# Attention and two gated layers on one core: products of zeros between the first real products, and a first group ordered by units

## The chip, the core and the metric

The kernel runs on one core of one Trainium2 chip. Its engines run side by side and meet at semaphores: PE (TensorE, matmuls and transposes), DVE (VectorE), ACT (ScalarE), POOL (GpSimd) and SP (SyncE, which here issues DMAs). The metric is the device time of one execution in microseconds, lower being better; a comparison takes the median of several executions.

## What is computed

The reference, cut to what matters (batch 2, 8 heads, 768 rows, head size 64):

```python
scores = scale * q @ k.T - slope[h] * dist      # keep: the first n_global=8 keys,
scores = where(keep, scores, -1e9)              #       and the last n_local=96 keys
a = softmax(scores);  x = a @ v                 # x: 2 x 768 x 512
h = relu(x @ w_in);   h = h * sigmoid(conv3(h)); x = h @ w_out
h = relu(x @ w_in2);  u, v = split(h);  v = normalise(v)
out = (u * (w_spatial @ v + b_spatial)) @ w_out2
```

Every matmul runs in 32-bit formats. The weight products behind attention are each made of three products of halves ("hi" and "lo"), which is why PE has so much to do there.

## The kernel before, in words

**Units.** Attention is cut into 48 units. A unit is 128 query rows of one pair of heads; three units of one pair are a triple p (`TG` = 3), four triples are a group (`GU` = 12 units), and there are four groups. Unit u needs, for each of its two heads, scores against 128 or 256 keys (128 for units 0, 3, 6, 9), and passes these steps:

1. PE `scores(p)` (L1426): the scores of the three units of triple p into PSUM; the third unit's are `third_scores`.
2. DVE `bias_scores(u)` (L1028): adds a bias table and takes the row minimum, two instructions of line L1038.
3. ACT `soften(u)` (L707): two exponentials, with the row sums.
4. DVE `invert_sums(u, n)` (L1044): adds a small number and takes the reciprocal, for n units at once (L1047, L1049).
5. POOL `scale_probs(u)` (L614): multiplies both heads' probabilities (L619).
6. PE `turn_probs(u)` (L1453): transposes (L1464).
7. ACT `copy_pt(u)` or DVE `take_pt(u)` (L1051): PSUM to SBUF; `turned_on_dve` (L403) says which.
8. PE `weigh(u)` (L1467): times the values (L1488). After a triple, ACT `round_x` and DVE `rest_of_x` take the result out of its bank, which the next triple's `weigh` waits for.

**Order.** No scheduler is involved: every engine runs its list in the order in which the program writes it. On PE a round is turn (three units), scores of the triple after next, weigh (three units). From triple 4 on, PE also runs the first weight layer of the group before (`f1`, L1509) between the transposes, 24 matmuls a triple. All the engines stand in strict lists, so an instruction whose semaphore is late holds everything behind it.

**What stands around the change.** PE begins with `WARM` = 10 products of a tile of zeros (L1515), then `scores(0)` and `scores(1)`. DVE builds three parts of the bias table on the way (`build_table`, L1013: one long and one short instruction each). Its inversions are made alone for units 0, 1, 2, 5, 8, 11, 14 and by pairs between. POOL also scales queries (L606, L600) and splits the first layer's weights into hi (L628) and lo (L630) in eight pieces (`PIECES_AFTER`).

Of the kernel before, what the change touches and what calls it, by code (L numbers as in the profile page):

```python
# [4 lines left out]
F32 = mybir.dt.float32  # L5
# [7 lines left out]
P = 128  # L13
# [16 lines left out]
WARM = 10  # L30
TW = 5 * P

# [35 lines left out]
PIECES_AFTER = {8: 1, 11: 1, 14: 2, 17: 2, 20: 2}  # L68
# [9 lines left out]
def build_program(nc, q, k0, k1, v0, v1, n_keys, weights, conv_w, b_spatial, out):  # L78
    ctx = ExitStack()
    with ctx:  # L80
# [205 lines left out]
        tables = sem("tables")  # L286
        path_in = sem("path_in")
# [115 lines left out]
        def turned_on_dve(u):  # L403
            return u < GU and (u % TG == 1 or u % TG == 2 and u // TG % 2 == 1)
# [21 lines left out]
        INVERTED_ALONE = (0, 1, 2, 5, 8, 11, 14)  # L426

        def inversion(u):
            if u < TG * (HP + 1):
                return sum(i <= u for i in INVERTED_ALONE) - 1 + sum(i <= u for i in range(TG, TG * (HP + 1), TG))  # L430
            return len(INVERTED_ALONE) + HP + u // TG - (HP + 1)

# [145 lines left out]
        def _(pool):  # L578
# [34 lines left out]

            def scale_probs(u):  # L614
# [26 lines left out]
            pieces = 0  # L641
            for u in range(ALL_UNITS):
# [8 lines left out]
                for _ in range(PIECES_AFTER.get(u, 0)):  # L651
                    split_piece(pieces)
                    pieces += 1
# [43 lines left out]
        def _(act):  # L697
# [88 lines left out]
            soften(0)  # L786
            soften(1)
            copy_pt(0)
            soften(2)
            for p in range(ALL_TRIPLES):  # L790
                u = TG * p
                for tt in range(TG):
                    if p + 1 < ALL_TRIPLES:
                        soften(u + TG + tt)
                    if p >= F1_FIRST and tt == 2:
                        relu_h(2 * (p - F1_FIRST))
                    if u + tt > 0 and not turned_on_dve(u + tt):
                        copy_pt(u + tt)
                    if tt == 0 and p > 0:
                        round_x(p - 1)  # L800
                if p >= F1_FIRST:
                    relu_h(2 * (p - F1_FIRST) + 1)
# [184 lines left out]
        def _(dve):  # L987
# [24 lines left out]

            def build_table(at_col, width):  # L1013
# [136 lines left out]
            build_table(AT_LATER, 2 * P)  # L1150
# [3 lines left out]
            take_pt(1)  # L1154
# [636 lines left out]
```

## Time and profile before

| | us |
|---|---|
| median of 3 runs | 373.0 |
| lowest and highest of them | 372.86, 374.86 |
| the profiled execution, its own time | 373.0 |
| its span, first to last instruction | 371.2 |
| PE busy in the span | 359.6 (97%) |
| DVE, ACT, POOL busy | 215.2, 176.8, 89.5 |

The profiled execution took 373.0 us in all, of which 371.2 us are the span; 1.8 us lie around it. Start times in the timeline count from the start of the span. A row "x12" stands for twelve instructions of one kind that follow each other, with their time together; the bracket behind it is the idle time of that engine just before, and what ended it. A score or weigh matmul of 32-bit data shows as two records, so a `scores` of three units with 12 records has 6 matmul instructions.

### The profile page before, as it was taken

Reading aid. Unit: us, or ns where it says so; the run is one execution under the profiler, and the core shown is the slowest. Engines: PE = TensorE matmul, PEld = TensorE weight load, DVE = VectorE, ACT = ScalarE, POOL = GpSimd, SP = SyncE. Lnnn points to the kernel's source line nnn. Section 1 sums busy time; section 2 is a strip of 40 time slices with the busy share of each in tenths; the row PEclk is TensorE's granted clock in tenths of the full one; section 3 lists DMA queues with packets and bytes.
Section 4 is the critical chain, followed back from the end, with each engine's and each line's share of the span. In section 5 each row is a group of like instructions: output and inputs, shape, how many; then the busy total and the mean of one; then the engine's idle time right before and its main releaser. Section 6 shows DMA issues by size and latency. Waiting matters only on the chain.

```text
span 371.2 us, 6142 instructions
## 1 busy us (share of the span) xinstructions
PE 359.6 (97%) x2266; PEld 326.4 (88%) x2266; DVE 215.2 (58%) x569; ACT 176.8 (48%) x448; POOL 89.5 (24%) x166
## 2 busy tenths in 40 slices
PE   6889999999999999999999999999999999999994
PEld 2557989888998999999989999998899999998883
DVE  6678599767867678779866780214863444440000
ACT  3577776666777579664364640213653111112221
POOL 4659986555443300000030200001400000000000
PEclk9699999999999999999999999999999999999999
DMA  7934332223422305322100000001241000002222
GB/s 223 398 136 128 94 95 78 81 94 96 141 82 63 130 0 171 98 74 64 49 2 0 3 0 0 2 0 45 69 158 58 0 2 0 0 2 86 86 87 91
DMA packets 12085, 27.70 MB, mean 75 GB/s; under 512 B 1552, under 2 KB 3984, under 8 KB 12048
## 3 DMA queue, kind: packets, MB, share of 16 engines
q1 hardware_dynamic: 11760, 27.10, 21.6%
q8 instruction: 20, 0.33, 0.4%
q14 instruction: 17, 0.14, 0.2%
q10 hardware_dynamic: 288, 0.13, 0.2%
HBM read 24.08 MB, written 3.15 MB: 73 GB/s over the span
## 4 chain that ended last, share of the span: by engine, by line
PE 93%; DVE 3%; POOL 1%; issue 1%; ACT 0%; DVEq 0%; POOLq 0%
PE bank L1538 20%; PE bank L1540 20%; PE bank L1539 19%; PE bank L1509 18%; PE bank L1464 6%; PE bank L1488 5%; PE bank L1419 5%; DVE p_sb L1038 1%; PE bank L1515 1%; POOL p_sb L619 1%; DVE pt_sb L1055 1%; DVE xT L1060 0%; POOL q_sb L600 0%; DVE denom L1049 0%; DVE denom L1047 0%
## 5 line engine op out<-in xcount | busy, mean ns | idle before, releaser
L1509 PE MATMUL bank<-xT,w_hi 128*128 128x384 f32 x256 | 69.4, 344 | 0.0
L711 ACT ACTIVATE p_sb<-p_sb,row_min 128x256 f32<-128x256 f32 (+1 forms) x96 | 46.3, 486 | 26.6 <-DVE row_min L1038 26.6
L619 POOL TENSOR_SCALAR p_sb<-p_sb,denom 128x256 f32<-128x256 f32 (+1 forms) x96 | 47.0, 504 | 47.2 <-DVE denom L1049 47.2
L1509 PEld LDWEIGHTS bank<-xT,w_hi 128*128 128x128 f32 x256 | 45.9, 188 | 0.2 <-issue 0.2
L1075 DVE SCALAR_TENSOR_TENSOR c_sb<-h_sb,conv_sb,c_sb 128x382 f32<-128x382 f32 (+1 forms) x64 | 43.0, 672 | 2.3
L1509 PE MATMUL bank<-xT,w_lo 128*128 128x384 f32 x128 | 44.1, 344 | 0.0
L1538 PE MATMUL bank<-g_hi,w_hi 128*128 128x386 f32 (+1 forms) x128 | 43.3, 338 | 0.0
L1540 PE MATMUL bank<-g_hi,w_lo 128*128 128x386 f32 (+1 forms) x128 | 43.2, 337 | 0.0
L1539 PE MATMUL bank<-g_lo,w_hi 128*128 128x386 f32 (+1 forms) x128 | 43.1, 336 | 0.0
L1038 DVE CUSTOM_DVE_ANT_0 p_sb<-bank,table 128x256 f32<-128x256 f32 (+1 forms) x96 | 32.6, 397 | 12.9 <-PE bank L1419 12.5
L635 POOL TENSOR_SCALAR rstd<-mean_var 128x1 f32<-128x1 f32 x12 | 4.5, 374 | 129.3 <-DVE mean_var L1103 129.3
L1464 PE MATMUL bank<-ident,p_sb 128*128 128x128 f32 x176 | 29.9, 286 | 4.1 <-POOL p_sb L619 4.0
L1540 PE MATMUL bank<-w_hi,vn 128*128 128x384 f32 x96 | 32.3, 336 | 0.0
L1538 PE MATMUL bank<-w_hi,vn 128*128 128x384 f32 x96 | 32.3, 336 | 0.0
L1539 PE MATMUL bank<-w_lo,vn 128*128 128x384 f32 x96 | 32.3, 336 | 0.0
L1464 PEld LDWEIGHTS bank<-ident,p_sb 128*128 128x128 f32 x176 | 20.6, 142 | 11.1 <-POOL p_sb L619 5.7
L775 ACT CAST gt<-u_sb 128x384 fp32r<-128x384 f32 x16 | 8.2, 513 | 42.8 <-DVE u_sb L1128 42.8
L719 ACT COPY pt_sb<-bank 128x512 f32<-128x512 f32 (+1 forms) x42 | 22.8, 543 | 7.6 <-PE bank L1464 6.9
L1419 PE MATMUL bank<-k_sb,q_sb 64*128 64x256 f32 (+1 forms) x192 | 25.6, 398 | 0.8 <-DMA k_sb<-in_k 0.6
L751 ACT ACTIVATE x<-bank 128x382 fp32r<-128x382 f32 (+1 forms) x16 | 7.9, 493 | 38.4 <-PE bank L1540 38.2
L1488 PEld LDWEIGHTS bank<-pt_sb,v_sb 128*64 128x64 f32 x352 | 19.2, 138 | 6.1 <-issue 4.8
L1539 PEld LDWEIGHTS bank<-g_lo,w_hi 128*128 128x128 f32 x128 | 24.2, 189 | 0.0
(93 smaller groups left out, 762.6 us busy)
## 6 DMA issues: line engine op xcount, KB each, us to landing
stage<-in_weights SPq DMA_DIRECT2D x17, 512.0 KB, 3.4
v_sb<-in_v SPq DMA_DIRECT2D x8, 390.0 KB, 3.6
k_sb<-in_k SPq DMA_DIRECT2D x8, 384.0 KB, 3.4
out_dram<-out_sb SPq DMA_DIRECT2D x12, 256.0 KB, 2.1
q_sb<-in_q SPq DMA_DIRECT2D x13, 192.0 KB, 2.4
v_sb<-in_v SPq DMA_DIRECT2D x6, 260.0 KB, 3.3
k_sb<-in_k SPq DMA_DIRECT2D x5, 256.0 KB, 2.9
stage_late<-in_weights SPq DMA_DIRECT2D x2, 512.0 KB, 10.7
```

Source lines behind the costliest of these rows:

```text
L619: nc.gpsimd.tensor_scalar(probs_h, probs_h, denom[:, u % SLOTS, h:h + 1], 1.0, ALU.mult, ALU.mult).then_inc(scaled, 1)
L711: nc.scalar.activation(p_sb[:, u % SLOTS, h, 0:n], p_sb[:, u % SLOTS, h, 0:n], ACT.Exp, bias=row_min[:, u % SLOTS, h:h + 1], scale=-1.0, a ...
L719: nc.scalar.copy(pt_sb[:, u % PT_SLOTS, :, 0:n], pt_ps(u)[:, :, 0:n]).then_inc(pt_in, 1)
L1038: nc.vector.tensor_tensor_reduce(out=p_sb[:, u % SLOTS, h, 0:n], in0=score_cols(u, h), in1=table[:, at_col:at_col + n], scale=slope(2 * hp ...
L1075: nc.vector.scalar_tensor_tensor(dst, src, w, dst, ALU.mult, ALU.add).then_inc(tapped, 1)
L1419: return nc.tensor.matmul(score_cols(u, h), queries[rows, tt * P:(tt + 1) * P], keys_t[rows, at_key:at_key + n], start=True, stop=True)
L1464: last = nc.tensor.transpose(pt_ps(u)[:, h, c:c + P], p_sb[:, u % SLOTS, h, c:c + P], ident[:])
L1488: last = nc.tensor.matmul(xt_ps[h * D:(h + 1) * D, tt * P:(tt + 1) * P], rows[:, h * DV:h * DV + D], pt_sb[:, u % PT_SLOTS, h, n * P:(n + ...
L1509: last = nc.tensor.matmul(h_bank(j)[:, 0:C], w, x, start=r == 0, stop=r == F1_GROUP - 1)
L1538: nc.tensor.matmul(ps, a_hi, b_hi, start=start, stop=False)
L1539: nc.tensor.matmul(ps, a_hi, b_lo, start=False, stop=False)
L1540: return nc.tensor.matmul(ps, a_lo, b_hi, start=False, stop=stop)
```

## The change

- **Products of zeros.** `WARM` becomes (8, 3, 6, 4): 8 products before `scores(0)`, 3 before `scores(1)`, 6 behind it, 4 behind the first turn. They write bank 4 and not bank 7.
- **The third table part.** Its long instruction leaves DVE; POOL makes it of two instructions, ahead of its first `scale_probs`, and DVE waits for it (`later_table`).
- **Copies.** In the first group only units 1, 4, 7, 10 are copied by DVE; units 5 and 11 go to ACT.
- **DVE by units.** In units 0 to 14 every inversion is alone. Ahead of the copy of unit u stands the inversion of unit u+2, behind it the biasing of unit u+4.
- **ACT by units.** `soften(2)` comes ahead of `copy_pt(0)`; in the first group `soften(u+3)` stands ahead of `copy_pt(u)` (behind it in triple 0).
- **POOL.** A piece of the weights is split in two steps: the rounding (L628 of before) of pieces 0 and 1 now stands behind units 6 and 9, the rest (L630 of before) still behind units 8 and 11.

```diff
-WARM = 10
+WARM = (8, 3, 6, 4)
+COUNT_STEPS = 5
-PIECES_AFTER = {8: 1, 11: 1, 14: 2, 17: 2, 20: 2}
+ROUND_AFTER = {6: 1, 9: 1, 14: 2, 17: 2, 20: 2}
+REST_AFTER = {8: 1, 11: 1, 14: 2, 17: 2, 20: 2}
...
         def turned_on_dve(u):
-            return u < GU and (u % TG == 1 or u % TG == 2 and u // TG % 2 == 1)
+            return u < GU and u % TG == 1
...
-        INVERTED_ALONE = (0, 1, 2, 5, 8, 11, 14)
+        ALONE = TG * (HP + 1)
...
+            later = table[:, AT_LATER:AT_T0]
+            pool.wait_ge(tables, COUNT_STEPS)
+            nc.gpsimd.tensor_scalar(later, rel[:, AT_LATER:AT_T0], count_f[:, 1:2], 1.0, ALU.is_ge, ALU.mult
+                                    ).then_inc(later_table, 1)
+            pool.wait_ge(later_table, 1)
+            nc.gpsimd.tensor_tensor(later, later, behind[:, AT_LATER:AT_T0], ALU.add).then_inc(later_table, 1)
...
             act.wait_ge(consts, 8)
-            soften(0)
-            soften(1)
-            copy_pt(0)
-            soften(2)
-            for p in range(ALL_TRIPLES):
+            for u in range(TG):
+                soften(u)
+            for u in range(GU):
+                if u < TG and not turned_on_dve(u):
+                    copy_pt(u)
+                soften(u + TG)
+                if u >= TG and not turned_on_dve(u):
+                    copy_pt(u)
+                if u % TG == 0 and u > 0:
+                    round_x(u // TG - 1)
+            for p in range(HP, ALL_TRIPLES):
...
             bias_scores(1)
             invert_sums(0, 1)
-            build_table(AT_LATER, 2 * P)
+            near = table[:, AT_LATER:AT_LATER + GK]
+            dve.wait_ge(later_table, 2)
+            link(nc.vector.tensor_tensor(near, near, reach[:], ALU.min))
             bias_scores(2)
             invert_sums(1, 1)
             bias_scores(3)
-            take_pt(1)
-            invert_sums(2, 1)
-            bias_scores(4)
-            bias_scores(5)
-            invert_sums(3, 2)
-            invert_sums(5, 1)
-            for p in range(1, ALL_TRIPLES + 1):
+            for u in range(GU):
+                invert_sums(u + 2, 1)
+                if turned_on_dve(u):
+                    take_pt(u)
+                if u % TG == 1 and u > TG:
+                    rest_of_x(u // TG - 1)
+                if u + 4 < ALONE:
+                    bias_scores(u + 4)
+            invert_sums(ALONE - 1, 1)
+            for p in range(HP, ALL_TRIPLES + 1):
...
+            def warm(n):
+                for _ in range(n):
+                    nc.tensor.matmul(banks[4][:], zeros[:, 0:P], zeros[:], start=True, stop=True)
+
+            warm(WARM[0])
             scores(0)
+            warm(WARM[1])
             scores(1)
+            warm(WARM[2])
...
                     turn_probs(TG * p + tt)
+                    if p == 0 and tt == 0:
+                        warm(WARM[3])
```

On PE, at the program's start, before (bank<-zeros are the products of zeros, k_sb,q_sb the scores, ident,p_sb the transposes):

```order
L1515 MATMUL bank<-zeros 128x512 x10
L1419 MATMUL bank<-k_sb,q_sb 128x128 x2
L1419 MATMUL bank<-k_sb,q_sb 128x256 x4
L1419 MATMUL bank<-k_sb,q_sb 128x128 x2
L1419 MATMUL bank<-k_sb,q_sb 128x256 x2
L1464 MATMUL bank<-ident,p_sb 128x128 x6
L1419 MATMUL bank<-k_sb,q_sb 128x256 x2
L1464 MATMUL bank<-ident,p_sb 128x128 x4
```

and now, of the same place:

```order
L1541 MATMUL bank<-zeros 128x512 x8
L1444 MATMUL bank<-k_sb,q_sb 128x128 x2
L1444 MATMUL bank<-k_sb,q_sb 128x256 x4
L1541 MATMUL bank<-zeros 128x512 x3
L1444 MATMUL bank<-k_sb,q_sb 128x128 x2
L1444 MATMUL bank<-k_sb,q_sb 128x256 x2
L1541 MATMUL bank<-zeros 128x512 x6
L1489 MATMUL bank<-ident,p_sb 128x128 x2
L1541 MATMUL bank<-zeros 128x512 x4
L1489 MATMUL bank<-ident,p_sb 128x128 x4
L1444 MATMUL bank<-k_sb,q_sb 128x256 x2
L1489 MATMUL bank<-ident,p_sb 128x128 x4
```

The real products keep their order; products of zeros stand in three places between them, 21 in all where there were 10.

On DVE, from the second half of the biasing of unit 3 on, before (a 128x128 or 256 ISA row with p_sb is a biasing, denom rows are an inversion, COPY is `take_pt(1)`):

```order
L1038 ISA p_sb,row_min<-bank,table 128x128
L1038 ISA row_min 128x1
L1055 COPY pt_sb<-bank 128x512
L1047 TENSOR_SCALAR denom<-denom 128x2
L1049 RECIPROCAL denom<-denom 128x2
```

and now:

```order
L1063 ISA p_sb,row_min<-bank,table 128x128
L1063 ISA row_min 128x1
L1072 TENSOR_SCALAR denom<-denom 128x2
L1074 RECIPROCAL denom<-denom 128x2
L1063 ISA p_sb,row_min<-bank,table 128x256
L1063 ISA row_min 128x1
L1063 ISA p_sb,row_min<-bank,table 128x256
L1063 ISA row_min 128x1
L1072 TENSOR_SCALAR denom<-denom 128x2
L1074 RECIPROCAL denom<-denom 128x2
L1080 COPY pt_sb<-bank 128x512
```

The copy of unit 1 now stands behind the inversions of units 2 and 3 and the biasing of unit 4.

On ACT, from its first exponential on, before (COPY is `copy_pt`, of unit 0 and then of unit 2):

```order
L711 ACTIVATE p_sb,denom<-p_sb,row_min 128x128 x2
L711 ACTIVATE p_sb,denom<-p_sb,row_min 128x256 x2
L719 COPY pt_sb<-bank 128x2x128
L711 ACTIVATE p_sb,denom<-p_sb,row_min 128x256 x2
L711 ACTIVATE p_sb,denom<-p_sb,row_min 128x128 x2
```

and now:

```order
L730 ACTIVATE p_sb,denom<-p_sb,row_min 128x128 x2
L730 ACTIVATE p_sb,denom<-p_sb,row_min 128x256 x4
L738 COPY pt_sb<-bank 128x2x128
L730 ACTIVATE p_sb,denom<-p_sb,row_min 128x128 x2
L730 ACTIVATE p_sb,denom<-p_sb,row_min 128x256 x2
```

The exponentials of unit 2 moved ahead of the copy of unit 0.

## Rows read from the trace of the kernel before

**Rows 1.** Page, part 2: PE's granted clock in 40 slices of the span, in tenths

```profile
PEclk9699999999999999999999999999999999999999
```

**Rows 2.** Waits of PE, whole span: us in total, times, longest

```profile
PE bank L1464 <- POOL p_sb L619: 4.0, 5, 1.3
```

**Rows 3.** Stages by windows: length, busy PE, PEld, DVE, ACT, POOL, clock, DMA, GB/s

```profile
0.00:34.50 34.50, 27.88 (x203) 16.89 (x203) 23.70 (x116) 20.13 (x72) 20.93 (x51) 0.90 0.63 222
34.50:371.20 336.70, 331.76 (x2066) 309.49 (x2064) 191.48 (x454) 156.68 (x377) 68.59 (x117) 1.00 0.18 60
```

**Rows 4.** Windows around the fall and rise of the clock

```profile
7.95:11.20 3.25, 0.76 (x4) 0.45 (x4) 2.64 (x16) 2.36 (x10) 1.58 (x4) 1.00 1.04 390
11.30:14.60 3.30, 2.73 (x12) 1.40 (x10) 2.35 (x11) 1.74 (x9) 1.62 (x4) 0.50 1.02 386
14.60:18.00 3.40, 3.40 (x20) 2.27 (x20) 1.20 (x9) 1.65 (x7) 2.80 (x7) 0.50 1.05 415
```

**Rows 5.** Timeline of the first 15 us: start, us, engine, line, instruction

```profile
4.26 0.39 PEld L1515 LDWEIGHTS bank<-zeros 128*128 128x128 bf16 x2 [0.28 <-issue]
...
5.07 1.36 PE L1419 MATMUL bank<-k_sb,q_sb 64*128 64x128 f32 x12
...
7.02 0.93 PE L1419 MATMUL bank<-k_sb,q_sb 64*128 64x128 f32 x8 [0.59 <-DMA k_sb<-in_k]
...
8.43 0.47 DVE L1015 SCALAR_TENSOR_TENSOR table<-rel,count_f,behind 128x256 f32<-128x256 f32 x1
...
8.61 0.87 POOL L619 TENSOR_SCALAR p_sb<-p_sb,denom 128x128 f32<-128x128 f32 x2 [2.64 <-DVE denom L1049]
...
9.28 0.58 PE L1464 MATMUL bank<-ident,p_sb 128*128 128x128 f32 x2 [1.33 <-POOL p_sb L619]
...
10.17 0.51 ACT L711 ACTIVATE p_sb<-p_sb,row_min 128x256 f32<-128x256 f32 x1
...
10.49 0.93 POOL L619 TENSOR_SCALAR p_sb<-p_sb,denom 128x256 f32<-128x256 f32 x2 [1.01 <-DVE denom L1049]
...
11.03 1.14 PE L1464 MATMUL bank<-ident,p_sb 128*128 128x128 f32 x4 [1.16 <-POOL p_sb L619]
...
11.40 0.58 POOL L606 TENSOR_SCALAR q_sb<-q_sb,q_scale 128x384 f32<-128x384 f32 x1
...
12.21 0.69 DVE L1055 COPY pt_sb<-bank 128x512 f32<-128x512 f32 x1 [1.34 <-PE bank L1464]
...
13.89 1.08 PE L1464 MATMUL bank<-ident,p_sb 128*128 128x128 f32 x4 [0.57 <-POOL p_sb L619]
...
14.90 2.51 PE L1419 MATMUL bank<-k_sb,q_sb 64*128 64x128 f32 x12
```

**Rows 6.** Timeline of the rounds behind it, 17 to 35 us

```profile
17.34 1.64 PE L1488 MATMUL bank<-pt_sb,v_sb 128*64 128x128 f32 x20
...
18.91 1.31 PE L1464 MATMUL bank<-ident,p_sb 128*128 128x128 f32 x10
...
21.72 0.55 DVE L1060 TENSOR_TENSOR xT<-bank,xT 128x384 fp32r<-128x384 f32 x1
...
22.32 1.31 PE L1488 MATMUL bank<-pt_sb,v_sb 128*64 128x128 f32 x20 [0.37 <-DVE xT L1060]
...
26.17 1.57 PE L1419 MATMUL bank<-k_sb,q_sb 64*128 64x256 f32 x12
...
26.41 1.28 POOL L630 TENSOR_TENSOR w_lo<-stage,w_hi 128x512 fp32r<-128x512 f32 x1
...
27.66 1.31 PE L1488 MATMUL bank<-pt_sb,v_sb 128*64 128x128 f32 x20
```

**Rows 7.** The last of these rounds, and the end of the stage

```profile
33.24 1.31 PE L1488 MATMUL bank<-pt_sb,v_sb 128*64 128x128 f32 x20
...
34.48 0.66 PE L1464 MATMUL bank<-ident,p_sb 128*128 128x128 f32 x4
```

**Rows 8.** Windows: the round from 27.6 us

```profile
27.60:33.20 5.60, 5.00 (x44) 3.15 (x42) 4.42 (x20) 4.21 (x15) 5.04 (x10) 1.00 0.36 107
```

More of the change, by code:

```diff
@@ L286, in build_program @@
         tables = sem("tables")
+        later_table = sem("later_table")
         path_in = sem("path_in")
@@ L423, in wait_chunk @@
                 eng.wait_ge(chunk_in[n % 2], 16 * (n // 2))
[L426 removed]
+        ALONE = TG * (HP + 1)
         def inversion(u):
[L429 to L431 removed]
+            return u if u < ALONE else ALONE + u // TG - (HP + 1)
         def values_of(u):
@@ L639, in invert_std @@
                                         ALU.pow).then_inc(rstd_in, 1)
-            pieces = 0
+            rounded = split = 0
             for u in range(ALL_UNITS):
@@ L650, in _ @@
                         scale_queries(pg)
-                for _ in range(PIECES_AFTER.get(u, 0)):
-                    split_piece(pieces)
-                    pieces += 1
+                for _ in range(ROUND_AFTER.get(u, 0)):
+                    round_piece(rounded)
+                    rounded += 1
+                for _ in range(REST_AFTER.get(u, 0)):
+                    rest_of_piece(split)
+                    split += 1
             for i in range(B * NT):
@@ L794, in _ @@
                         soften(u + TG + tt)
-                    if p >= F1_FIRST and tt == 2:
+                    if tt == 2:
                         relu_h(2 * (p - F1_FIRST))
-                    if u + tt > 0 and not turned_on_dve(u + tt):
-                        copy_pt(u + tt)
-                    if tt == 0 and p > 0:
+                    copy_pt(u + tt)
+                    if tt == 0:
                         round_x(p - 1)
-                if p >= F1_FIRST:
-                    relu_h(2 * (p - F1_FIRST) + 1)
+                relu_h(2 * (p - F1_FIRST) + 1)
             round_x(ALL_TRIPLES - 1)
@@ L1164, in _ @@
                         bias_scores(u + TG + tt)
-                    if tt > 0 and p < HP and turned_on_dve(u + tt):
-                        take_pt(u + tt)
                 rest_of_x(p - 1)
@@ L1513, in _ @@
             pe.wait_ge(consts, 1)
-            for _ in range(WARM):
-                nc.tensor.matmul(banks[7][:], zeros[:, 0:P], zeros[:], start=True, stop=True)
+            def warm(n):
+                for _ in range(n):
+                    nc.tensor.matmul(banks[4][:], zeros[:, 0:P], zeros[:], start=True, stop=True)
+            warm(WARM[0])
             scores(0)
+            warm(WARM[1])
             scores(1)
+            warm(WARM[2])
             pe.wait_ge(consts, 9)
```

23 lines of the change are left out of this document (12 added, 11 removed).

## Prediction, made before the changed kernel ran

> **What bounds the kernel now.** I began with the windows by stage. From 34.5 us to the end PE is busy 331.76 of 336.70 us; in the 34.5 us before it, 27.88, with a granted clock of 0.90 [rows 3]. The page shows the clock below its level in the second slice alone, apart from the 9 of the first [rows 1]. So there are two kinds of time: 336.7 us that only less work on PE could shorten, and a first stage of 34.5 us with 6.6 us of idle PE and some us at half clock. The list of PE's waits says what the idle time is: 4.0 us in five waits of a transpose for POOL's scaling, the end of the chain scores, bias, exponential, inversion, scaling [rows 2]. The change touches this stage alone, so the question is when PE reaches the point where it no longer waits: the turn of unit 12, at 34.48 us [rows 7]. What arrives earlier there ends earlier.
>
> The clock: between the second scores and 11.2 us PE is busy 0.76 of 3.25 us, the granted clock still 1.00. In the 3.30 us behind it the clock is 0.50, and also in the 3.40 us after those [rows 4]. These are the two levels, 2.4 and 1.2 GHz. The fall follows a stretch in which PE did little: it waited 1.33 us, worked 0.58, waited 1.16 [rows 5]. Half clock shows in the durations: 12 score records take 2.51 us at 14.90 [rows 5] and 1.57 at 26.17, where four of them are longer too [rows 6].
>
> **The start (-0.4 us).** Two products of zeros fewer stand ahead of `scores(0)`. The last two weight loads of zeros take 0.39 us together [rows 5], so `scores(0)` can begin 0.4 us before 5.07. If its operands were late the gain would be 0; I take 0.4. `scores(1)` still begins at 7.02, since a transfer of keys released it [rows 5]. The 3 products ahead of it fit: scores(0) ends 0.4 us before 6.43, and three cost 0.6 us by the pair of 0.39.
>
> **The third table (-0.5 us on DVE's chain).** The 0.47 us at 8.43 leave DVE, between the first inversion and the biasing of unit 2 [rows 5]. POOL gets two instructions. Neither is in the trace; the first is bounded below by a scaling of 256 columns (half of 0.93 for two, 0.47 [rows 5]) and the second lies between half and the whole of the 1.28 us for 512 columns [rows 6]. That is 1.1 to 1.8 us, and POOL has 2.64 us idle just ahead of its first scaling [rows 5]; with the 0.9 us by which that scaling may come earlier, at worst 0.1 us is left. Cost taken: 0. Inversion(1) and so POOL's scaling of unit 1 move from 10.49 to 9.6, by 0.4 + 0.5.
>
> **The products of zeros behind scores(1) and turn(0).** At 0.2 us each, 6 last 1.3 us from 7.02 + 0.8, to 9.1, and turn(0) began at 9.28 [rows 5]. The 4 last 0.85 us behind it: turn(0) at 9.1 takes 0.25, so they end at 10.2; turn(1) can begin at 9.6 + 0.54 = 10.15 (POOL's start to PE's, 10.49 to 11.03 [rows 5]). They fill the gaps and cost 0 to 0.3 us; I take 0. With them PE is busy nearly throughout 7.0 to 10.6, where it had been busy for a quarter. I therefore take the clock at 1.00 throughout.
>
> **Turn(2): from 13.89 to 11.6.** Before, the exponentials of unit 2 began at 10.17, behind a copy that waited for turn(0). Its inversion stood behind `take_pt(1)`, 12.21 to 12.90, which had waited 1.34 us for turn(1) [rows 5]. Both orders are gone. What is late next is POOL: scaling of unit 1 from 9.6 (0.93), scaling of queries (0.58 at 11.40), first half of unit 2 (0.5) [rows 5]: 11.6 us. The inversion is ready before: biasing of unit 2 ends at 9.2, two exponentials of 0.5 and the inversion at 10.6.
>
> **Weigh(0): from 17.34 to 13.5.** Before, 3.45 us from turn(2) to it at half clock (13.89, 14.90, 17.34 [rows 5, 6]). At full clock: turn(2) 0.7, held by POOL's second half (0.46), and 12 score records at half of the spacing 17.34 - 14.90, so 1.2. Sum 11.6 + 0.7 + 1.2 = 13.5. That is 3.8 us gained.
>
> **The three rounds: from 15.90 to 13.7.** From weigh(0) to weigh(9) PE took 33.24 - 17.34 = 15.90 us, in rounds of 4.98, 5.34 and 5.58 [rows 6, 7]. Its own work in a round is 33.24 to 34.48 = 1.24 for weigh [rows 7], 1.31 less the tail for the turn, and 1.49 for scores (26.17 to 27.66 [rows 6]): 4.0 us. After the change the inversions are one unit apart, so the turn is fed early; the late one is the biasing of the round's last unit, which the third scores wait for and which now stands behind `take_pt` and `rest_of_x`. That loop: weigh 1.24, turn of the first unit 0.25 and second 0.5, result out 0.2, copy 0.6, `rest_of_x` 0.46, biasing 0.75 (0.69 and 0.55 are the full lengths [rows 5, 6], of which 0.1 overlaps the next), third scores 0.5, semaphores 0.1: 4.6 us. Three: 13.8, less 0.1 since the first round's short unit makes its scores shorter. Two copies less on DVE (1.4 us) and four inversions more (0.28 each, 1.1) cancel; ACT gets the two copies and had 4.21 of 5.60 us busy [rows 8].
>
> POOL is the engine near its bound: 5.04 of 5.60 us [rows 8], with a piece of weights in a round. At 5.1 us it is slower than a round of 4.6. Splitting the piece puts 0.6 us behind unit 6 and 1.28 behind unit 8. POOL begins this at 15.5 (scaling of unit 6), so two rounds bring it to 25.7 + 0.8 for unit 12, needed at 28.4. The cover is 1.4 to 1.9 us. Were it gone, each further 0.1 us on POOL would be one on PE.
>
> **Sum.** Turn(12) begins at 13.5 + 13.7 + 1.24 = 28.4 instead of 34.48: 6.1 us. From there on the order is the same, and PE has no wait behind 34.5 us: of the 336.70 us with 331.76 busy, the rest is the end of the program [rows 3]. The profiled execution took 373.0 us, equal to the median of the three, so **373.0 - 6.1 = 366.9 us**. Bounds of this case: the rounds' own work instead of 4.6 would give 4.0, 1.4 us less after half-filled gaps, 365.5; products of zeros that hold turns by 0.3, late operands 0.4 and rounds of 4.9 give 368.5.
>
> **A rule against this change.** Rows first: at 11.3 to 14.6 us PE was busy 2.73 of 3.30 us, 8 transposes among it, and the clock stayed at 0.50 until 18 [rows 4]. The Trainium skill, "TensorE: Matmul & The Clock Gate", Part 4, says that a transpose does not count as PE being busy in the same way. The row agrees, though it does not prove it. By that rule a tighter first group, in which transposes are a third of PE's work, could still lose the clock; the rounds at 19 to 34 us ran at 1.00 with the same share [rows 1], which speaks against it.
>
> **Rivals.**
> 1. *The zeros do not hold the clock* and it falls as before, for 6.8 us. Then 2.4 us of PE's work there take twice their time where PE is the late one (turn(2) to weigh(0) 1.5 us, the turn and scores behind it 1.7): 3.2 us of the gain go, 370.1. For: the idle stretches of 0.3 to 0.9 us ahead of third scores remain. Against: PE is filled where it was empty.
> 2. *Given back later*: weights or POOL late for the first layer, so that PE waits behind 28 us. POOL's cover is 1.4 us and four pieces stand behind unit 14 (3.8 us); PE does not need them before turn(15), 8.6 us later. It would take a loss of 4.5 us to come to 371.4 to 374. Nothing shows it.
> 3. *Slower: the clock falls at about 14 us, in rounds whose third is transposes, and stays at half until the first layer's dense products.* Three rounds with 4.0 us of PE's work take 8.0 instead of 4.6, 10.2 us more than 366.9: 377.1. It decides when half clock lasts longer than about two rounds (3.4 us each). Against: the rows of 19 to 34 us at full clock.
>
> **Chances.** Forecast 0.80 (365.5 to 368.5), rival 1 0.11, rival 2 0.05, rival 3 0.04. The range takes in the first two: 365.3 to 370.6. A measurement of this kernel can tell some 0.5% from no change, 1.9 us: faster is below 371.1. Faster 0.90, same 0.05, slower 0.05.
>
> **What would show it.** Right: the clock row without the dip; turn(2) at 11.6, weigh(0) at 13.5, weigh(9) near 27.2, turn(12) at 28.4; among PE's waits third scores for a biasing, about 0.5 us a round; POOL's wait of 4.0 us down to about 1; all behind turn(12) 6 us earlier and alike. Wrong: a clock below 1.00 between 11 and 28 us; a wait of PE behind 30 us; a transpose that waits for POOL by over 0.5 us in the rounds, which would make POOL the bound.

## Result, and the profile after

| | before | after |
|---|---|---|
| median (us) | 373.44 (4 runs, 372.86 to 374.86) | 368.55 (4 runs, 367.51 to 369.05) |
| ratio of after to before | | 0.986 (0.982 to 0.990) |
| profiled execution, its own time | 373.0 | 368.85 |
| its span | 371.2 | 367.0 |
| `turn(12)` begins in the span | 34.48 | 30.69 |

The change makes the kernel 1.4% faster. The forecast was 366.9 us and the range 365.3 to 370.6: sign and range hold, and the gain between the two profiled executions is 4.15 us where 6.1 were expected (4.9 between the medians). The median lies just above the forecast's own bounds, 365.5 to 368.5. Nearly two fifths of the time that was expected at `turn(12)` is missing, and the missing part is what the experiments are about.

The page of after, busy time and then busy tenths and the granted clock in 40 slices, answers to [rows 1]:

```profile
PE 359.4 (98%) x2277; PEld 326.0 (89%) x2277; DVE 215.2 (59%) x574; ACT 178.1 (49%) x450; POOL 91.1 (25%) x168
...
PE   8989999999999999999999999999999999999995
...
PEclk9999999999999999999999999999999999999999
```

The clock row has lost its dip. The windows of after, at the times of [rows 3, 4, 8] (length, busy PE, PEld, DVE, ACT, POOL, granted clock, DMA share, GB/s):

```profile
0.00:34.50 34.50, 31.34 (x237) 20.08 (x238) 27.60 (x131) 24.80 (x87) 28.37 (x61) 1.00 0.67 239
...
7.95:11.20 3.25, 3.14 (x17) 1.21 (x14) 2.80 (x18) 2.42 (x10) 1.36 (x4) 1.00 1.05 403
11.30:14.60 3.30, 3.24 (x24) 1.81 (x22) 2.61 (x14) 2.79 (x12) 2.89 (x8) 1.00 1.04 393
14.60:18.00 3.40, 3.40 (x40) 2.65 (x38) 3.04 (x14) 2.96 (x12) 2.77 (x7) 1.00 1.04 401
27.60:33.20 5.60, 5.13 (x49) 4.07 (x45) 4.81 (x24) 4.17 (x15) 5.60 (x11) 1.00 0.32 108
```

PE is busy 3.14 of 3.25 us where it had been busy 0.76, and the clock stands at 1.00 in the two stretches where [rows 4] have 0.50. POOL, with 20.93 us busy in the first 34.5 [rows 3], now has 28.37, and 5.60 of 5.60 in the last window. The waits of PE over the whole span (total, times, longest), against [rows 2]:

```profile
PE bank L1444 <- DVE row_min L1063: 1.6, 3, 0.7
PE bank L1541 <- POOL zeros L582: 1.3, 1, 1.3
PEld bank L1489 <- POOL p_sb L630: 2.1, 9, 0.4
```

PE's 4.0 us of waiting for POOL are gone from its matmuls; 1.6 us of third scores for a biasing have come. The second row is the wait for the tile of zeros at the program's start, which before has as well. The third says that the weight loads of the transposes (PEld) still wait for POOL, 2.1 us in nine waits of at most 0.4, where before has

```profile
PEld bank L1464 <- POOL p_sb L619: 5.7, 17, 1.4
```

The timeline of after at the places of [rows 5 to 7] (start, us, engine, line, instruction):

```profile
1.30 3.59 PE L1541 MATMUL bank<-zeros 128*128 128x512 bf16 x8 [1.30 <-POOL zeros L582]
...
4.82 1.83 PE L1444 MATMUL bank<-k_sb,q_sb 64*128 64x128 f32 x12
...
5.75 1.15 POOL L620 TENSOR_SCALAR table<-rel,count_f 128x256 f32<-128x256 f32 x1
...
6.99 0.87 POOL L623 TENSOR_TENSOR table<-table,behind 128x256 f32<-128x256 f32 x1
7.32 0.60 DVE L1042 TENSOR_TENSOR table<-table,reach 128x32 f32<-128x32 f32 x1
7.33 0.93 PE L1444 MATMUL bank<-k_sb,q_sb 64*128 64x128 f32 x8
8.09 0.42 DVE L1063 CUSTOM_DVE_ANT_0 p_sb<-bank,table 128x256 f32<-128x256 f32 x1 [0.17 <-DVE table L1042]
...
9.77 0.58 PE L1489 MATMUL bank<-ident,p_sb 128*128 128x128 f32 x2
...
10.10 0.16 DVE L1072 TENSOR_SCALAR denom<-denom 128x2 f32<-128x2 f32 x1
...
11.09 0.89 PE L1489 MATMUL bank<-ident,p_sb 128*128 128x128 f32 x4
...
12.65 0.80 PE L1489 MATMUL bank<-ident,p_sb 128*128 128x128 f32 x4
...
14.67 1.31 PE L1513 MATMUL bank<-pt_sb,v_sb 128*64 128x128 f32 x20
...
18.85 0.70 PE L1444 MATMUL bank<-k_sb,q_sb 64*128 64x256 f32 x4 [0.68 <-DVE row_min L1063]
...
24.18 1.31 PE L1513 MATMUL bank<-pt_sb,v_sb 128*64 128x128 f32 x20
24.59 0.94 POOL L630 TENSOR_SCALAR p_sb<-p_sb,denom 128x256 f32<-128x256 f32 x2
25.09 0.47 DVE L1072 TENSOR_SCALAR denom<-denom 128x2 f32<-128x2 f32 x1
...
25.42 1.85 PE L1489 MATMUL bank<-ident,p_sb 128*128 128x128 f32 x10
...
25.85 0.94 POOL L630 TENSOR_SCALAR p_sb<-p_sb,denom 128x256 f32<-128x256 f32 x2 [0.32 <-DVE denom L1074]
...
29.44 1.31 PE L1513 MATMUL bank<-pt_sb,v_sb 128*64 128x128 f32 x20
...
30.69 0.66 PE L1489 MATMUL bank<-ident,p_sb 128*128 128x128 f32 x4
```

Three things are to be seen.

- **The start is late.** `scores(0)` takes 1.83 us where [rows 5] have 1.36 for the same 12 records, and the 8 products of zeros ahead take 0.45 us each where those behind it take 0.25 (1.47 us for 6): PE ran at half clock until about the middle of `scores(0)`. This is read from the durations alone, since the granted clock of the first windows is written as 1.00 in both kernels.
- **The table's minimum takes 0.60 us.** L1042 has 32 columns. It begins at 7.32 and ends at 7.92, as POOL's L623 ends (6.99 + 0.87 = 7.86). The biasing of unit 1 waits for it.
- **The additions take up to 0.47 us.** L1072 adds a small number to 128x2 elements. The one at 25.09 ends at 25.56, as POOL's scaling ends (24.59 + 0.94 = 25.53). This instruction ends with POOL, not after a time of its own. So do the seven others that took 0.27 us or more: each ends some 0.02 to 0.04 us behind a POOL instruction.

The second and the third look like one mechanism, which the experiments put to the test: a small DVE instruction with its data in SBUF waits until the POOL instruction in flight is done. By group, over 8 to 34.5 us of after (busy us, mean ns):

```profile
L1072 DVE TENSOR_SCALAR denom<-denom 128x2 f32<-128x2 f32 x15 | 4.1, 271 | 0.5 <-ACT p_sb L730 0.4
```

0.16 us is what one takes while POOL is idle (those at 8.78 and 10.10), so 15 x (0.271 - 0.16) = 1.7 us of DVE's time go there, most of it in the rounds. It reaches PE in two ways: DVE's list runs later, and with it the biasing that the third scores wait for; and the inversion is late for POOL. The second is seen in the third round: the addition at 25.09 belongs to unit 11, POOL stands idle for 0.32 us ahead of that unit's scaling at 25.85, and the turn takes 1.85 us where the turn of the second round takes 1.31.

### The profile page after: what moved, and what is told of

It is laid out like the page before. It is cut to its first block, busy times and chain, and to the rows that moved or that the text cites. A ratio compares the mean times of both kernels' runs of the same rounds, so it can differ in the third digit from the quotient of the medians.

```text
span 367.0 us, 6173 instructions
## 1 busy us (share of the span) xinstructions
PE 359.4 (98%) x2277; PEld 326.0 (89%) x2277; DVE 215.2 (59%) x574; ACT 178.1 (49%) x450; POOL 91.1 (25%) x168
## 4 chain that ended last, share of the span: by engine, by line
PE 96%; DVE 2%; issue 1%; ACT 0%; POOL 0%; DVEq 0%; POOLq 0%
PE bank L1570 20%; PE bank L1572 20%; PE bank L1571 20%; PE bank L1534 18%; PE bank L1444 6%; PE bank L1489 5%; PE bank L1513 5%; PE bank L1541 2%; DVE p_sb L1063 1%; DVE xT L1085 0%; DVE denom L1072 0%; DVE pt_sb L1080 0%; ACT out_sb L801 0%; POOL zeros L582 0%; DVE denom L1074 0%
## 5 line engine op out<-in xcount | busy, mean ns | idle before, releaser
L630 POOL TENSOR_SCALAR p_sb<-p_sb,denom 128x256 f32<-128x256 f32 (+1 forms) x96 | 47.1, 508 | 42.9 <-DVE denom L1074 42.9
L1100 DVE SCALAR_TENSOR_TENSOR c_sb<-h_sb,conv_sb,c_sb 128x382 f32<-128x382 f32 (+1 forms) x64 | 41.7, 651 | 2.3
L1489 PE MATMUL bank<-ident,p_sb 128*128 128x128 f32 x176 | 28.1, 279 | 0.3
L738 ACT COPY pt_sb<-bank 128x512 f32<-128x512 f32 (+1 forms) x44 | 23.9, 544 | 7.9 <-PE bank L1489 7.4
L1145 DVE TENSOR_TENSOR t<-bank,bsp 128x384 f32<-128x384 f32 x16 | 8.9, 558 | 26.1 <-PE bank L1572 26.1
```

The lines of the kernel that those rows point to most:

```text
L630: nc.gpsimd.tensor_scalar(probs_h, probs_h, denom[:, u % SLOTS, h:h + 1], 1.0, ALU.mult, ALU.mult).then_inc(scaled, 1)
L738: nc.scalar.copy(pt_sb[:, u % PT_SLOTS, :, 0:n], pt_ps(u)[:, :, 0:n]).then_inc(pt_in, 1)
L1100: nc.vector.scalar_tensor_tensor(dst, src, w, dst, ALU.mult, ALU.add).then_inc(tapped, 1)
L1489: last = nc.tensor.transpose(pt_ps(u)[:, h, c:c + P], p_sb[:, u % SLOTS, h, c:c + P], ident[:])
```

## Experiments

`turn(12)`, `weigh(0)` and the rounds (from `weigh(0)` to `weigh(9)`) are of the profiled execution, the medians of all its runs; an interval is that of the ratio to before, at 95%. Each ratio is to executions of before made beside that kernel. Their median was 372.62 us for `zeros_only`, `order_only`, `accum_sum` and `table_on_dve` and 373.44 to 373.47 for the others, so kernels of these two groups are compared by their ratios and not by their medians. "Then" is the time from the end of `scores(0)` to `weigh(0)`.

| kernel | median | ratio | `scores(0)` takes | then | `weigh(0)` | rounds | `turn(12)` |
|---|---|---|---|---|---|---|---|
| before | 373.44 | 1 | 1.36 | 10.91 | 17.34 | 15.90 | 34.48 |
| after | 368.55 | 0.982 to 0.990 | 1.83 | 8.02 | 14.67 | 14.77 | 30.69 |
| `zeros_only` | 370.05 | 0.991 to 0.996 | 1.36 | 9.24 | 15.11 | 15.56 | 31.91 |
| `order_only` | 371.11 | 0.992 to 0.997 | 1.36 | 10.20 | 16.68 | 15.33 | 33.25 |
| `accum_sum` | 367.11 | 0.982 to 0.987 | 1.36 | 7.64 | 13.64 | 14.10 | 28.99 |
| `table_on_dve` | 368.84 | 0.987 to 0.992 | 1.72 | 8.19 | 14.74 | 14.77 | 30.75 |
| `after_again` | 368.63 | 0.984 to 0.990 | 1.73 | 8.11 | 14.66 | 14.76 | 30.66 |
| `stt_sum` | 367.88 | 0.982 to 0.988 | 1.46 | 7.59 | 13.87 | 14.65 | 29.77 |
| `accum_bias_first` | 367.15 | 0.980 to 0.985 | 1.98 | 8.00 | 14.80 | 12.89 | 28.97 |
| `round_late` | 368.30 | 0.982 to 0.989 | 2.22 | 8.02 | 15.06 | 14.52 | 30.82 |
| `all_three` | 367.07 | 0.980 to 0.986 | 1.50 | 7.61 | 13.93 | 13.02 | 28.20 |
| `ten_first` | 369.56 | 0.985 to 0.991 | 2.09 | 7.61 | 15.38 | 14.78 | 31.40 |
| `copies_back` | 368.69 | 0.983 to 0.990 | 1.62 | 7.63 | 14.07 | 14.83 | 30.14 |

### The zeros alone, and the order alone

`zeros_only` is before with the four groups of zeros; `order_only` is after with the old ten.

```diff
-WARM = 10
+WARM = (8, 3, 6, 4)
```

> The kernel before with the products of zeros alone (8, 3, 6, 4); every other order is that of before. If the clock is held by them (theory): the granted clock is 1.00 throughout, scores and transposes of 11 to 18 us take half their time, the turn of unit 12 starts near 32.2 us instead of 34.5, time about 2.3 us below before, some 371.0. If the zeros only fill idle time and the unit order does the work (rival): the clock falls as before, time that of before, 373.4.

```diff
-WARM = (8, 3, 6, 4)
+WARM = (10, 0, 0, 0)
```

> The changed kernel with the ten products of zeros of before, all ahead of the first scores; the other orders as changed. Theory (two parts that add roughly): the clock falls near 11 us and rises some 7 us later, rounds as in the changed kernel; turn of unit 12 near 33 us, time 371 to 372. Rival (the earlier units fill PE enough by themselves): no fall of the clock, time as the changed kernel, 368.5.

Windows of `order_only`, around the fall of the clock:

```profile
7.95:11.20 3.25, 0.81 (x4) 0.48 (x4) 2.89 (x19) 2.54 (x10) 1.48 (x4) 1.00 1.02 381
11.30:14.60 3.30, 3.29 (x13) 1.87 (x14) 2.58 (x13) 1.81 (x9) 2.25 (x7) 0.50 1.02 388
14.60:18.00 3.40, 3.40 (x24) 2.57 (x24) 1.07 (x7) 2.09 (x9) 1.68 (x4) 0.50 1.04 411
```

and of `zeros_only`:

```profile
7.95:11.20 3.25, 2.93 (x15) 1.29 (x13) 2.12 (x13) 2.37 (x11) 2.13 (x5) 1.00 1.02 386
11.30:14.60 3.30, 2.21 (x19) 1.44 (x20) 2.70 (x13) 1.98 (x9) 1.27 (x4) 1.00 1.05 402
14.60:18.00 3.40, 3.38 (x38) 2.37 (x34) 2.32 (x12) 2.79 (x12) 2.89 (x7) 1.00 1.04 402
```

The zeros alone decide the clock. With them and the old order it stays at 1.00; without them and with the new order it falls, after a stretch with PE busy 0.81 of 3.25 us, and stays at half for 3.30 us in which PE is busy 3.29. `turn(12)` comes 2.57 us earlier by the zeros alone (34.48 to 31.91), 1.23 us by the order alone (to 33.25), and 3.79 us by both. That they add up so exactly is luck, since executions of nearly the same program differ by 0.55 us at this place (after and `copies_back` below); in the medians they add up too, within the noise: 0.7% and 0.6% alone, 1.4% together. In the rounds the zeros alone save 0.34 us of 15.90 and the order alone 0.57, though its first round still begins at half clock (`weigh(0)` takes 2.01 us instead of 1.31); both together save 1.13, where 2.2 were expected.

### The addition in the form that also writes a sum

If the additions wait because of the way this DVE instruction reads SBUF, another form of it should not wait.

```diff
-nc.vector.tensor_scalar(sums, sums, 1e-9, None, ALU.add)
+nc.vector.tensor_scalar(sums, sums, 1e-9, 0.0, ALU.add, ALU.add, accum_out=count_f[:, 5:6])
```

> The changed kernel with one edit: the addition ahead of a reciprocal also writes out its accumulator, so that it is another form of the same instruction. Theory (DVE's addition waits for the POOL instruction in flight): the additions, 0.16 to 0.47 us in the changed kernel, take at most 0.2 us, the three rounds 14.8 us shrink to about 14.0, the turn of unit 12 starts 0.7 to 1.0 us earlier, 367.6. Rival (the rounds are long for other reasons, the durations only show a queue): the additions stay long, or shorten and the rounds stay 14.8 us, 368.5.

The group of the additions in `accum_sum`, and the timeline at the place of the addition that had taken 0.47 us:

```profile
L1072 DVE TENSOR_SCALAR_CACHE_REDUCE denom<-denom 128x2 f32<-128x2 f32 x14 | 2.1, 151 | 0.6 <-ACT p_sb L730 0.5
```

```profile
24.24 1.54 PE L1490 MATMUL bank<-ident,p_sb 128*128 128x128 f32 x10
...
24.36 0.93 POOL L630 TENSOR_SCALAR p_sb<-p_sb,denom 128x256 f32<-128x256 f32 x2
24.94 0.15 DVE L1072 TENSOR_SCALAR_CACHE_REDUCE denom<-denom 128x2 f32<-128x2 f32 x1
```

At 24.94 it begins while POOL scales, until 25.29, and takes 0.15 us: it waits for nothing. The mean goes from 271 to 151 ns and the rounds from 14.77 to 14.10. The rounds are now 4.68, 4.68 and 4.74 us; the prediction had 4.6. The third, which was 5.26, brings 0.52 of the 0.67 us: its turn takes 1.54 us instead of 1.85, and its third scores wait 0.26 instead of 0.47. That is the mechanism shown for the rounds. The 1.03 us at `weigh(0)` are not its doing: this execution had an early rise of the clock (`scores(0)` at 4.64, 1.36 us, so its end is 0.65 us earlier), and at 6.70 the table's minimum fell beside POOL's other table instruction and took 0.19. The times of the whole kernel don't show the gain by themselves: the ratios are 0.985 and 0.986, and `stt_sum` below, whose additions wait, has 0.985 as well.

The Trainium skill, "SBUF — State Buffer", "Who interferes with whom", says that DVE and GpSimd share a pair of SBUF ports as an exclusive lock, held for the whole instruction, and that `tensor_scalar`, though not the form that also writes out its accumulator, can run in a two-port mode that takes it. The rows agree: up to 0.47 us in the plain form, 0.15 in the other. The prediction had not drawn on this rule.

### The addition with two operands in SBUF

```diff
-nc.vector.tensor_scalar(sums, sums, 1e-9, None, ALU.add)
+nc.vector.scalar_tensor_tensor(sums, sums, 1e-9, sums, ALU.add, ALU.max)
```

> The changed kernel with the addition ahead of the reciprocal written as an instruction with two inputs, both the same sums in SBUF: (s + 1e-9) max s. If DVE and POOL meet at DVE's second read of SBUF (theory), it waits for the POOL instruction in flight as the plain addition does: durations up to 0.5 us, rounds 14.8 us, 368.5. If only the plain one-input form is affected (rival), durations stay under 0.25 us, rounds 14.1 us, 367.5.

Timeline of `stt_sum`:

```profile
23.72 0.93 POOL L630 TENSOR_SCALAR p_sb<-p_sb,denom 128x256 f32<-128x256 f32 x2
24.21 0.44 DVE L1072 SCALAR_TENSOR_TENSOR denom<-denom 128x2 f32<-128x2 f32 x1
```

It again ends with POOL (24.65 both), so the plain form isn't the only one that waits. The Trainium skill, "SBUF — State Buffer", "Who interferes with whom", names DVE instructions with two SBUF inputs too, against a GpSimd instruction that reads SBUF; the row agrees. Another row of the same trace does not: the minimum L1042 has two inputs in SBUF and L620 reads SBUF, and yet L1042 takes 0.19 us at 6.95, in the middle of L620 (6.01 to 7.16). It is the same in `accum_sum` and `all_three`. Here the measurement decides; POOL's spans in a profile are rough, by its own legend, and the cause is open. The rounds are 14.65, almost those of after, which says once more that what shortened them in `accum_sum` was the additions that no longer wait. `weigh(0)` is 0.80 us earlier, `scores(0)` having taken 1.46 instead of 1.83 us and the minimum 0.19 instead of 0.60.

### The third table back on DVE, and after once more

```diff
-            nc.gpsimd.tensor_scalar(later, rel[:, AT_LATER:AT_T0], count_f[:, 1:2], 1.0, ALU.is_ge, ALU.mult
-                                    ).then_inc(later_table, 1)
...
-            nc.gpsimd.tensor_tensor(later, later, behind[:, AT_LATER:AT_T0], ALU.add).then_inc(later_table, 1)
...
+build_table(AT_LATER, 2 * P)
```

> The changed kernel with the third table part built on DVE again, as before. By the prediction's sum this costs 0.5 us: 369.0. By the theory that POOL's two instructions hold up DVE's short minimum (0.60 us instead of 0.2) and so the biasing of unit 1, about 0.4 us come back and the two nearly cancel: the biasing of unit 1 starts 0.4 us earlier, that of unit 2 within 0.1 us of the changed kernel, time 368.4 to 368.7.

> The changed kernel itself once more, as the measure for the runs beside it: 368.5 us. If the clock of PE rises earlier in this execution, before the first scores, they take 0.9 us instead of 1.8 and the turn of unit 12 starts up to 0.7 us earlier than in the first profile (30.7 us); the three rounds stay 14.8 us either way.

Timeline of `table_on_dve`, the places of 7.32, 8.09 and 9.41 in after:

```profile
7.21 0.19 DVE L1036 TENSOR_TENSOR table<-table,reach 128x32 f32<-128x32 f32 x1
...
7.58 0.42 DVE L1057 CUSTOM_DVE_ANT_0 p_sb<-bank,table 128x256 f32<-128x256 f32 x1 [0.17 <-DVE table L1036]
...
8.55 0.47 DVE L1034 SCALAR_TENSOR_TENSOR table<-rel,count_f,behind 128x256 f32<-128x256 f32 x1
...
9.46 0.42 DVE L1057 CUSTOM_DVE_ANT_0 p_sb<-bank,table 128x256 f32<-128x256 f32 x1 [0.17 <-DVE table L1036]
```

With POOL's two instructions gone, the minimum takes 0.19 us instead of 0.60 and the biasing of unit 1 begins 0.51 us earlier; the 0.47 us of the long instruction are back behind it, and the biasing of unit 2 begins at 9.46 where after has 9.41. Against this execution of after the two cancel to 0.05 us. `after_again` is like after: the minimum takes 0.70 us, the clock rises no earlier (`scores(0)` 1.73 us), and `turn(12)` is at 30.66.

Whether DVE is held here isn't fixed, however. It is held if its table instructions fall beside POOL's L623. In `copies_back`, which differs from after only in who copies units 5 and 11, the minimum starts ahead of L623:

```profile
7.11 0.19 DVE L1042 TENSOR_TENSOR table<-table,reach 128x32 f32<-128x32 f32 x1
...
7.21 0.73 POOL L623 TENSOR_TENSOR table<-table,behind 128x256 f32<-128x256 f32 x1
...
8.79 0.42 DVE L1063 CUSTOM_DVE_ANT_0 p_sb<-bank,table 128x256 f32<-128x256 f32 x1 [0.17 <-DVE table L1177]
```

The biasing of unit 2 then begins 2.35 us behind the end of `scores(0)`, where after has 2.76 and `table_on_dve` 2.91: 0.56 us are gained, as forecast. Of the ten traces with the table on POOL, five, this one among them, are not held ("then" 7.6 us in the table) and four, after among them, are (8.0 to 8.1; in `round_late` it is L1040 that meets L623 and takes 1.03 us instead of 0.48). The tenth is `order_only`, which is held too: the minimum takes 0.65 us. So in one half of the executions seen this part of the change gains nothing, since what it takes from DVE's list comes back as a wait of DVE for POOL, and in the other half it gains half a microsecond. The ratios lean the same way, 0.990 for `table_on_dve` against 0.986 and 0.987 for after, but their intervals overlap.

### The biasing ahead of the copy

The third scores wait for the biasing of the round's last unit, which stands behind `take_pt` and `rest_of_x`. This kernel has the accumulator form and the biasing first.

```diff
                 invert_sums(u + 2, 1)
+                if u + 4 < ALONE:
+                    bias_scores(u + 4)
                 if turned_on_dve(u):
                     take_pt(u)
                 if u % TG == 1 and u > TG:
                     rest_of_x(u // TG - 1)
-                if u + 4 < ALONE:
-                    bias_scores(u + 4)
```

> The changed kernel with the accumulator form of the addition, and on DVE the biasing of unit u+4 ahead of the copy of unit u and of the rest of x. Theory (the loop over the third scores is what is left of the rounds): PE's wait for the biasing of a round's last unit, 1.3 us in all, goes; a shorter wait for the copy or the rest of x takes its place; the three rounds shrink from 14.1 to about 13.2 us, time 366.2. Rival (POOL is the bound, 5.1 us of work in a round with a weight piece): the waits move to transposes that wait for POOL and the rounds stay at 14 us, 367.1.

PE in `accum_bias_first`, one round:

```profile
21.60 1.57 PE L1445 MATMUL bank<-k_sb,q_sb 64*128 64x256 f32 x12
23.09 1.64 PE L1514 MATMUL bank<-pt_sb,v_sb 128*64 128x128 f32 x20
...
24.07 0.42 PEld L1514 LDWEIGHTS bank<-pt_sb,v_sb 128*64 128x64 f32 x8 [0.35 <-ACT pt_sb L738]
```

The 12 records of scores are one block without a wait, and the rounds fall by 1.21 us against `accum_sum`, to 12.89. What is late next is ACT's copy, 0.35 us in a `weigh`. So the loop named in the prediction (weigh, turn, result out, copy, `rest_of_x`, biasing, third scores) did set the rounds, and POOL, the rival, did not. In `turn(12)` the gain hardly shows, 28.97 against 28.99, because this execution began late (`weigh(0)` at 14.80 instead of 13.64). The times show it beside `after_again`, which is of the same group: 366.26 to 367.18 us in five runs against 368.11 to 369.40 in four, for the accumulator form and the new order together. The 366.2 that were expected were not reached.

### Where POOL rounds the weights

```diff
-ROUND_AFTER = {6: 1, 9: 1, 14: 2, 17: 2, 20: 2}
+ROUND_AFTER = {8: 1, 11: 1, 14: 2, 17: 2, 20: 2}
```

> The changed kernel with each of the first two weight pieces rounded behind units 8 and 11 again, right ahead of its rest, 1.9 us in one piece on POOL. If splitting the piece matters: the scaling of unit 9 or 12 comes 0.6 us later relative to PE and the third round grows by 0.3 to 0.6 us, 369.0. If POOL's slack hides it: rounds 14.8 us, 368.5.

Timeline of `round_late`, the additions that took 0.32 us at 18.71 and 0.47 at 25.09 in after:

```profile
19.09 0.17 DVE L1072 TENSOR_SCALAR denom<-denom 128x2 f32<-128x2 f32 x1
...
25.47 0.17 DVE L1072 TENSOR_SCALAR denom<-denom 128x2 f32<-128x2 f32 x1
```

I had expected that splitting the piece helps or does nothing; without the split the rounds are 0.25 us shorter (14.52 against 14.77), nearly all of it in the third (5.02 against 5.26). In after the first of the two additions waits for the rounding itself (L642, 18.39 to 19.01), and the second begins in the second half of a scaling pair (24.59 to 25.53). With the rounding moved, both take 0.17 us and the third turn 1.60 instead of 1.85; other additions still wait (0.37 us at 21.55, 0.43 at 26.51). A miss: the split of the piece costs a little, by the same mechanism. The medians of `round_late` and `after_again`, 368.30 and 368.63, are too close to show it, with runs from 367.15 to 369.45 in the one.

### The three together

> The changed kernel with three edits: the accumulator form of the addition, the biasing of unit u+4 ahead of the copy of unit u, and the first two weight pieces rounded behind units 8 and 11. If the third round's 0.25 us, which the late rounding gained beside the changed kernel, are POOL's and add to the other two: rounds 12.6 to 12.7 us (12.9 without it), 366.7. If they only came from the additions that waited for POOL (rival), the accumulator form has taken them already: rounds 12.9, 367.0.

This is `accum_bias_first` with `round_late`. The median is 367.07, as the rival expected. The rounds are 13.02, no shorter than without `round_late` (12.89): once the additions wait for nothing, rounding later gains nothing. `turn(12)` is the earliest of all, 28.20, and yet the span is 365.4 us, against 365.3 in `accum_bias_first` with 28.97. PE keeps what it gained until its end: the last copy of the output begins 0.79 us earlier. Timelines of `accum_bias_first` and `all_three` at the end:

```profile
360.80 0.59 ACT L801 COPY out_sb<-bank 128x512 f32<-128x512 f32 x1 [2.21 <-PE bank L1573]
```

```profile
360.01 0.58 ACT L801 COPY out_sb<-bank 128x512 f32<-128x512 f32 x1 [2.21 <-PE bank L1573]
```

From this copy to the end of the span it is 4.5 us in the one and 5.4 in the other. In all thirteen traces it is 4.3 to 5.4 us, while from `turn(12)` to this copy it is 331.8 to 332.0 us in every one. The output's last transfer thus makes single executions differ by up to 1.1 us at their very end, whatever was gained ahead of it; why it does was not settled.

### Ten products of zeros first

```diff
-WARM = (8, 3, 6, 4)
+WARM = (10, 3, 6, 4)
```

> The changed kernel with 10 products of zeros ahead of the first scores and not 8. Theory (the clock rises when it rises, 4.2 to 5.9 us into the span in the executions so far, and not after a number of products): scores(0) starts 0 to 0.4 us later than 4.82 and runs at full clock more often; weigh(0) at 14.5 to 14.9, within 0.3 us of the changed kernel, 368.5. Rival (8 products are too few to bring the clock up in time): scores(0) takes 1.36 us, weigh(0) at 14.0, 368.0.

Two more products ahead of `scores(0)` do not bring the clock's rise forward, and both expectations for `weigh(0)` (14.5 to 14.9, and 14.0) and for the time were missed. All ten ran at half clock, `scores(0)` began at 5.68 instead of 4.82 and still took 2.09 us, and `weigh(0)` came 0.71 us later than in after. In the executions with 8 or 10 products the rise came anywhere from ahead of `scores(0)` to late in it (12 such records take 1.36 us at full and 2.51 at half clock [rows 5]), so it doesn't follow their number. With 8 products the first weight load of `scores(0)` is released by the transfer of its keys, at 4.5 to 4.8 us; products that last beyond that only push the scores back.

### Units 5 and 11 copied by DVE again

```diff
-            return u < GU and u % TG == 1
+            return u < GU and (u % TG == 1 or u % TG == 2 and u // TG % 2 == 1)
```

> The changed kernel with the copies of units 5 and 11 on DVE again. The prediction held that 1.4 us less on DVE and four more inversions cancel. If DVE's list is what the rounds hang on: each of the two copies stands ahead of the biasing of units 9 and 15, rounds 15.0 to 15.5, 368.9. If ACT's list is as full (rival): no difference, 14.8, 368.5.

Rounds 14.83 against 14.77, median 368.69 against 368.55: no difference, as the rival said. DVE has the time for these two copies, and they don't stand in the loop that sets the rounds. Yet this execution has `weigh(0)` at 14.07, 0.60 us ahead of after: 0.21 by the end of `scores(0)`, and 0.4 because the table instructions were not held, as shown above.

## Why the prediction was right, and where it was short

| | forecast | after |
|---|---|---|
| `scores(0)` begins | 4.7 | 4.82 |
| `turn(0)` | 9.1 | 9.77 |
| `turn(1)` | 10.15 | 11.09 |
| `turn(2)` | 11.6 | 12.65 |
| `weigh(0)` | 13.5 | 14.67 |
| three rounds | 13.7 | 14.77 |
| `turn(12)` | 28.4 | 30.69 |

**What bounds the kernel: right.** After `turn(12)` nothing changed: 331.8 us to the last copy of the output before, 332.0 after, and 331.8 to 332.0 in every kernel. What arrived earlier there came earlier to that copy; behind it the end varies by 1.1 us.

**The clock: right.** It stays at 1.00 (the 9 of the first slice in [rows 1] was no exception, 9 being the highest digit), and `order_only` and `zeros_only` show that it is the zeros that hold it. Rival 1 (zeros don't hold the clock) and rival 3 (half clock until the first layer) fall with that, and rival 2 (given back later) with the 332.0 us above; the 3.8 us in it are the price of two weight pieces and not of four. The products themselves cost nothing, as taken: `turn(1)` begins 0.53 us behind POOL's scaling at 10.56, where the prediction had 0.54. The range was wide enough partly because it took in rival 1: the median, 368.55, lies just above the bounds that the forecast had by itself. The transposes, a third of PE's work in the rounds, did not bring the clock down either, so the rule against the change had no effect here. Rival 1's price for the fall, 3.2 us, is somewhat above what the zeros measure: 2.57 us with the old order, 30.69 against 33.25 = 2.56 with the new.

**The start: -0.4 forecast, +0.2 measured at the end of `scores(0)`.** Before, `scores(0)` ended at 6.43, and now at 6.65. Its start gained 0.25 us of the 0.4, the keys' transfer releasing it at 4.82, and its duration was taken from [rows 5] at 1.36. It took 1.83, because the clock rose later in this execution. The term that failed is the constant duration: among the kernels with 8 zeros it is 1.36 to 2.22 us. Of the 1.17 us that `weigh(0)` is late, 0.12 are the start of `scores(0)`, 0.47 its duration and 0.41 the table's minimum (next paragraph); 0.17 are spread over the rest. `accum_sum`, which had the 1.36 and a minimum that was not held, has `weigh(0)` at 13.64, beside the 13.5 forecast. The step from scores to `weigh` was therefore sized right, for an execution with an early rise and no such wait.

**The third table: -0.5 forecast, 0 in this execution, -0.56 in others.** The two POOL instructions were bounded at 1.1 to 1.8 us and took 2.02. That was still covered: at 7.86 they are done, and the first scaling begins at 9.25 behind its inversion, not behind them. The step that failed is "cost taken: 0": it looked at POOL's list alone and asked whether POOL had the time, not what DVE would meet while POOL worked. The minimum of 32 columns waited 0.4 us, and `table_on_dve` shows that this and the saving cancel. `copies_back` shows the forecast's 0.5 where the minimum is not held.

**The three rounds: 13.7 forecast, 14.77 measured.** The loop was named rightly, as `accum_bias_first` shows, and the waits of the third scores are 0.68, 0.45 and 0.47 us against about 0.5. The term that was mis-sized is "two copies less on DVE and four inversions more (0.28 each) cancel". An inversion is 0.28 us only while POOL is quiet. Before, POOL was quiet because it was itself waiting for that inversion: [rows 5] have it idle for 2.64 and 1.01 us ahead of its scalings. Working by units feeds POOL early, and then it is in flight when more than half of the additions come: eight of the fifteen took 0.27 us or more. The other half of that term, the copies, is worth next to nothing by `copies_back`. The trace of before shows the price once, beside the 1.28 us of POOL at 26.41 [rows 6], which end at 27.69:

```profile
27.13 0.58 DVE L1047 TENSOR_SCALAR denom<-denom 128x4 f32<-128x4 f32 x1
```

Four elements in 0.58 us, where its neighbours take 0.14 to 0.24: this row was there to be read.

With additions that wait for nothing the rounds are 14.10. The 0.4 us left to 13.7 are rounds of 4.68, 4.68 and 4.74 where 4.5, 4.6 and 4.6 were taken: 0.1 us a round on the loop, and a first round that its short unit did not shorten. What makes these was not looked into.

**POOL near its bound: right as far as it went.** PE's wait for POOL was expected at about 1 us. It is gone from the matmuls, and 2.1 us of short waits are left with the weight loads of the transposes. The cover was worked out for unit 12 and held there. At unit 11 it did not: the third turn takes 1.85 us instead of 1.31. Of these 0.54 us, 0.31 came by way of DVE's addition, and 0.23 stay in `accum_sum`, where POOL has no gap ahead of this scaling.

**Together**: 1.17 us late at `weigh(0)` and 1.07 us in the rounds make 2.24 of the 2.29 us missing at `turn(12)`. The forecast of 366.9 is near what `accum_sum` comes to (367.11), which has the early start, a minimum that is not held and no waiting additions. Part of that nearness is luck: `turn(12)` is at 28.99 there and not at 28.4, and its group has the lower times, of before as well.

## What to carry to other kernels

A gap on PE that stands ahead of a fall of the clock is worth filling with products of zeros; here what they gave and what a better order gave added up within the noise. When an order is tightened, an engine that used to be quiet is now in flight next to its neighbour: for DVE and POOL, look for small DVE instructions with data in SBUF whose ends coincide with the ends of POOL's, before and after, and price them at up to the length of POOL's instruction. Where one stands in the chain that matters, a form that doesn't wait (here the one that also writes a sum) is a cure of one line, worth 0.67 us of the rounds; putting the biasing ahead of the copy was worth another 1.21. And a change of less than 1 us can't be told from two single executions.

## What the runs showed that I had not expected

- **A DVE instruction of two columns can take 0.47 us beside POOL and 0.16 without**, so its size says nothing of its price. It wasn't a matter of form alone: L1042, two inputs in SBUF, took 0.60 us beside POOL's L623, which has two inputs, and 0.19 us in `accum_sum` beside POOL's L620, which has one (5.92 to 7.08, L1042 at 6.70). Why the one holds it and the other seems not to is open.
- **POOL's comparison (`is_ge`, then a product) of 256 columns took 1.15 us**, a product by a column of as many 0.48 (before, at 3.69).
- **The start and the end of the program vary at equal code.** With 8 products of zeros ahead, `scores(0)` ended at 6.00 to 7.04 us, and a wait of DVE for POOL of 0.4 us came or did not; together they moved `weigh(0)` by up to 1.4 us. The end varies by 1.1 us. Two kernels compared by one execution each can differ by that much, in either direction, for these reasons alone.
- **PE at 1.2 GHz stayed there while busy 3.29 of 3.30 us** (`order_only`, 11.3 to 14.6), with all of it real work.
